# Retention, routing and a bilinear layer on one core: x rows by one-pass transposes, logits in four 32-column groups, another order of the window branches

## The reference

```python
# attention: a decaying state, 4 batches x 8 heads x 768 positions x 64
for t in range(S):
    state = gamma * state + k[t] v[t]^T
    y[t] = scale * q[t] @ state
x = y as 3072 rows of 512
# mixture of 8 experts, one per token
logits = x @ w_gate + modality_bias[modality_id]
e_idx = argmax(logits); gate_w = softmax(logits)[e_idx]
out[rows of e] = gate_w * (relu(x @ w1[e]) @ w2[e])        # 512 -> 1024 -> 512
# bilinear layer
h = (x @ wa) * (x @ wb)        # 512 -> 1024
out = (h @ w3) @ w_out         # the kernel forms wc = w3 @ w_out once
```

## Time and profile before

| what | value |
|---|---|
| median of 3 runs | 903.04 us (902.85 to 903.64) |
| the profiled execution | 903.01 us, of which its span 901.3 us |
| PE busy | 863.3 us (96% of the span) |
| PE weight loads busy | 739.7 us (82%) |
| DVE, ACT, POOL busy | 32%, 29%, 9% |
| mean granted clock of the core | 0.989 |

### The profile page before, as it was taken

The page is one execution under the profiler, slowest core; times in us unless marked ns, Lnnn a source line. Parts: engine busy times, 40 slices in busy tenths (PEclk is TensorE's granted clock), DMA queues, the critical chain, the costliest instruction groups (busy, mean ns, idle before and its releaser), DMA issues.

```text
span 901.3 us, 13561 instructions
## 1 busy us (share of the span) xinstructions
PE 863.3 (96%) x5236; PEld 739.7 (82%) x5237; DVE 286.2 (32%) x495; ACT 258.8 (29%) x460; POOL 85.5 (9%) x106
## 2 busy tenths in 40 slices
PE   6999999599999999999998999999999999999995
PEld 5888878488999998888888788888888888888884
DVE  2566679531212234121227231121221230230210
ACT  2445533231222233121326222222221221231210
POOL 1222002202020120202000001001001001001001
PEclk9999999889999999999999999999999999999998
DMA  9999751313120343202145102002002002001000
GB/s 326 373 334 363 288 211 47 143 40 103 47 93 0 93 169 110 60 33 55 38 143 184 47 1 82 12 1 82 12 0 81 12 0 93 0 0 47 1 13 35
DMA packets 44006, 84.97 MB, mean 94 GB/s; under 512 B 7744, under 2 KB 8256, under 8 KB 43968
## 3 DMA queue, kind: packets, MB, share of 16 engines
q1 hardware_dynamic: 33376, 60.33, 19.0%
q0 software_dynamic: 4736, 14.72, 5.1%
q10 hardware_dynamic: 5856, 9.40, 3.0%
HBM read 63.42 MB, written 21.00 MB: 94 GB/s over the span
## 4 chain that ended last, share of the span: by engine, by line
PE 91%; DVE 3%; issue 2%; DMA 1%; ACT 1%; ACTq 1%; POOL 0%; DVEq 0%
PE bank L382 79%; PE pair L754 3%; PE bank L771 3%; PE bank L744 2%; PE pair L832 1%; DMA mbias<-n_moe_modality_bias_dram 1%; PE bank L762 1%; PE bank L783 1%; PE bank L884 1%; ACT xTu L553 0%; DVE we_p L953 0%; DVE w3T L953 0%; ACTq L337 0%; DVE prob L971 0%; ACT we_p L553 0%
## 5 line engine op out<-in xcount | busy, mean ns | idle before, releaser
L382 PE MATMUL bank<-yT,wab 128*128 128x512 f32 x1152 | 262.2, 389 | 2.0 <-issue 2.0
L382 PEld LDWEIGHTS bank<-yT,wab 128*128 128x128 f32 x1152 | 216.2, 188 | 47.0 <-issue 2.2
L382 PE MATMUL bank<-xT,we_p 128*128 128x512 f32 (+2 forms) x768 | 153.6, 360 | 13.3 <-issue 10.5
L382 PEld LDWEIGHTS bank<-xT,we_p 128*128 128x128 f32 x768 | 135.4, 191 | 30.9 <-issue 11.8
L382 PE MATMUL bank<-hT,we_p 128*128 128x512 f32 (+2 forms) x768 | 153.6, 357 | 0.0
L382 PEld LDWEIGHTS bank<-hT,we_p 128*128 128x128 f32 x768 | 132.9, 188 | 14.6
L382 PE MATMUL bank<-wc,gT 128*128 128x512 f32 x576 | 131.5, 389 | 0.0
L382 PEld LDWEIGHTS bank<-wc,gT 128*128 128x128 f32 x576 | 108.1, 188 | 22.4
L1232 DVE TENSOR_TENSOR g<-bank,acopy 128x512 f32<-128x512 f32 x48 | 33.2, 692 | 259.1 <-PE bank L382 259.1
L1193 DVE SCALAR_TENSOR_TENSOR hT<-bank,hT 128x512 fp32r<-128x512 f32 x64 | 44.1, 691 | 172.4 <-ACT hT L632 172.4
L632 ACT ACTIVATE hT<-bank 128x512 fp32r<-128x512 f32 x64 | 38.2, 598 | 114.9 <-PE bank L382 114.9
(11 more groups left out here) (144 smaller groups left out, 545.3 us busy)
## 6 DMA issues: line engine op xcount, KB each, us to landing
we_raw<-in_moe_w_dram SPq DMA_DIRECT2D x6, 2048.0 KB, 9.2
yT_sorted<-yout ACTq DMA_DIRECT2D x8, 1024.0 KB, 4.4
qkv<-in_q_t_dram SPq DMA_DIRECT2D x24, 256.0 KB, 3.9
qkv<-in_v_dram SPq DMA_DIRECT2D x24, 256.0 KB, 5.5
x_rows<-x_keep SPq DMA_DIRECT2D x24, 256.0 KB, 5.5
ytile<-yT_sorted SPq DMA_DIRECT2D x6, 1024.0 KB, 5.0
qkv<-in_k_t_dram SPq DMA_DIRECT2D x23, 256.0 KB, 5.3
qkv<-in_k_dram SPq DMA_DIRECT2D x20, 256.0 KB, 5.9
```

The costliest lines, as they stand in the source:

```text
L382: i = pe.matmul(out_, left(a), right(b), start=(first and n == 0), stop=(last and n == 2), **kw)
```

## The change

PE no longer multiplies by `iw`. It transposes `xTu` in four one-pass transposes against the identity (`rows`, L756), and forms the logits transposed (`gates`, L762): the weights are 32 columns of a padded gate matrix, one group of 32 output partitions for each of the four feature parts. ACT copies this 128 by 128 block (`lTu`), PE transposes it (`logit_rows`, L768), DVE sums the four parts, a unit later than before. The features stand in two neighbouring PSUM banks (`attn`), so that one ACT operation of 512 columns copies them. The state update runs a unit late, behind the next unit's scores. `c_ident` is no longer loaded to `iw`, and the wait for three small transfers becomes one for the gate weights. Twelve of the sixteen `w3` pieces are loaded after the last unit's set. The branches of the window loop are written widest first.

```diff
-            act.dma_start(iw[:, :, 0:P], c_ident.unsqueeze(1).to_broadcast([P, KD, P])).then_inc(s_gatew, 16)
-            act.dma_start(iw[:, :, P:XW], w_gate.rearrange("(c p) e -> p c e", p=P)).then_inc(s_gatew, 16)
+            act.wait_ge(s_zero, 2)
+            act.dma_start(w_gate_t[:, :, 0:E], w_gate.rearrange("(c p) e -> p c e", p=P)).then_inc(s_gatew, 16)
...
             def keep(u):
-                act.wait_ge(s_lg, u + 1)
+                act.wait_ge(s_xl, u + 1)
+                copy(lTu[:, :], pair[:, 0:1, P:2 * P].rearrange("p a t -> p (a t)")).then_inc(s_gt, 1)
                 dst = x_keep[:, u, :]
                 copy(dst.rearrange("p (j t) -> p j t", j=KD), pair[:, :, 0:P]).then_inc(s_keep, 1)
...
-                for odd in range(2):
-                    for r in range(2):
-                        rows = slice((r ^ odd) * D, (r ^ odd) * D + D)
-                        i = copy(xTu[rows, odd:KD:2, :], bank[5 - r][rows, :].rearrange("p (j t) -> p j t", j=KD)[:, odd:KD:2, :])
-                i.then_inc(s_xTu, 1)
+                copy(xTu[:, :, :], attn[:, :, 0:2 * P].rearrange("p r (m t) -> p r m t", m=2)).then_inc(s_xTu, 1)
...
-            def rows_and_logits(u, first):
-                if first:
-                    pe.wait_ge(s_gatew, 48)
+            def rows(u):
                 pe.wait_ge(s_xTu, u + 1)
-                if not first:
+                if u:
                     pe.wait_ge(s_keep, u)
+                    pe.wait_ge(s_lg, u)
                 for j in range(KD):
-                    i = pe.matmul(pair[:, j, 0:XW], xTu[:, j, :], iw[:, j, :], start=True, stop=True, skip_group_check=True)
+                    pe.transpose(pair[:, j, 0:P], xTu[:, j, :], ident)
+
+            def gates(u):
+                if u == 0:
+                    pe.wait_ge(s_gatew, 16)
+                for j in range(KD):
+                    i = pe.matmul(pair[j * SQ:(j + 1) * SQ, 0, P:2 * P], w_gate_t[:, j, :], xTu[:, j, :], start=True, stop=True, skip_group_check=True)
                 i.then_inc(s_xl, 1)
+
+            def logit_rows(u):
+                pe.wait_ge(s_gt, u + 1)
+                pe.wait_ge(s_keep, u + 1)
+                pe.transpose(pair[:, 2, P:2 * P], lTu[:, :], ident).then_inc(s_lt, 1)
...
             def unit(c, b, u):
                 scores(c, b, u, u == 0)
+                if 0 < u <= NT - B:
+                    update((b - 1) % B, u - 1, u <= B)
+                if u == 1:
+                    pe.wait_ge(s_const, 16)
                 if u:
-                    rows_and_logits(u - 1, u == 1)
+                    rows(u - 1)
+                    gates(u - 1)
                 if c:
                     from_state(b, u)
                 from_chunk(c, b, u, c == 0)
-                if c < C - 1:
-                    update(b, u, c == 0)
+                if u:
+                    logit_rows(u - 1)
...
-            w3_product(0, {2: lambda: rows_and_logits(NT - 1, False)})
+            w3_product(0, {1: last_rows, 4: lambda: logit_rows(NT - 1)})
...
-                with pe.If(size < 3):
-                    wide(2)
-                with pe.If(size > 2):
-                    with pe.If(size < 4):
+                with pe.If(size > 3):
+                    wide(4)
+                with pe.If(size < 4):
+                    with pe.If(size > 2):
                         wide(3)
-                    with pe.If(size > 3):
-                        wide(4)
+                    with pe.If(size < 3):
+                        wide(2)
...
             def unit(c, b, u):
+                if u > 1:
+                    keep_logits(u - 2)
                 masked(u)
-                if u:
-                    keep_logits(u - 1)
+                if 0 < u <= NT - B:
+                    if u == 1:
+                        dve.wait_ge(s_const, 16)
+                    new_state((u - 1) // B, (b - 1) % B, u - 1)
```

More of the change, by code:

```diff
@@ L15 @@
 from contextlib import ExitStack
+import itertools
 import numpy as np
@@ L50, in build @@
     RANKED = 4
+    SQ = 32
     XCH = 16
@@ L114, in build @@
         ident = sm["ident"]
-        XW = P + E
-        iw = fixed("iw", [P, KD, XW])
+        w_gate_t = fixed("w_gate_t", [P, KD, SQ])
         logits = fixed("logits", [P, E, NT])
@@ L148, in build @@
         xTu = r("xTu", [P, KD, P])
+        lTu = r("lTu", [P, P])
         x_keep = region(at_i)("x_keep", [P, NT, DM])
@@ L209, in build @@
         assert top[0] <= nc.sbuf_usable_end, (top[0], nc.sbuf_usable_end)
-        bank = [ctx.enter_context(nc.psum_tensor(f"bank{i}", [P, BANK], F32)) for i in range(6)]
+        bank = [ctx.enter_context(nc.psum_tensor(f"bank{i}", [P, BANK], F32)) for i in range(4)]
+        attn = ctx.enter_context(nc.psum_tensor("attn", [P, 2, BANK], F32))
+        bank += [attn[:, i:i + 1, :].rearrange("p a w -> p (a w)") for i in range(2)]
         pair = ctx.enter_context(nc.psum_tensor("pair", [P, KD, BANK // 2], F32))
@@ L238, in build @@
         s_xl = sem("s_xl")
+        s_gt = sem("s_gt")
+        s_lt = sem("s_lt")
         s_lg = sem("s_lg")
@@ L422, in sp_unit @@
                     sp.dma_start(w_out_raw[:, n:n + 1, :], wo_src[:, n:n + 1, :]).then_inc(s_wor[n], 16)
-                if B + KF <= u < C * B:
+                if B + KF <= u < 2 * B + KF:
                     w3_load(u - B - KF)
-                    if c == C - 1:
-                        w3_load(u - B - KF + B)
             each_unit(sp_unit)
+            for n in range(B, 2 * KF):
+                w3_load(n)
             for u in range(NT - LAG, NT - 1):
@@ L490, in _ @@
             pool.memset(zero[:, :], 0.0).then_inc(s_zero, 1)
+            pool.memset(w_gate_t[:, :, :], 0.0).then_inc(s_zero, 1)
             pool.wait_ge(s_const, 16)
@@ L761, in from_state @@
                     for r in range(2):
-                        pe.matmul(bank[5 - r][out_rows(j, r), j * P:(j + 1) * P], state[head_rows(r), b, j, :], qdk[head_rows(r), b % 2, j, :],
+                        pe.matmul(attn[out_rows(j, r), r, j // 2 * P:(j // 2 + 1) * P], state[head_rows(r), b, j, :], qdk[head_rows(r), b % 2, j, :],
                                   start=(j < 2), stop=False, skip_group_check=True)
@@ L770, in from_chunk @@
                         h = 2 * j + r
-                        i = pe.matmul(bank[5 - r][out_rows(j, r), j * P:(j + 1) * P], qkv[:, b, V, h * D:(h + 1) * D], prob[:, r, j, :],
+                        i = pe.matmul(attn[out_rows(j, r), r, j // 2 * P:(j // 2 + 1) * P], qkv[:, b, V, h * D:(h + 1) * D], prob[:, r, j, :],
                                       start=(first and j < 2), stop=(j >= HP - 2), skip_group_check=True)
@@ L821, in counts, with last_rows @@
                 pe.matmul(bank[7][:, 0:E * NT], sm["ones"], chosen, start=True, stop=True).then_inc(s_cnt, 1)
-            w3_product(0, {2: lambda: rows_and_logits(NT - 1, False)})
+            def last_rows():
+                rows(NT - 1)
+                gates(NT - 1)
+            w3_product(0, {1: last_rows, 4: lambda: logit_rows(NT - 1)})
             def x_rows(w, chunks):
@@ L939, in biases @@
             def biases():
-                dve.wait_ge(s_gatew, 48)
-                dve.wait_ge(s_mod, 16)
+                dve.wait_ge(s_mod, 32)
                 link(dve.tensor_copy(modf[:, :], mod_i[:, :, 0:1].rearrange("p n a -> p (n a)")))
@@ L974, in keep_logits @@
             def keep_logits(u):
-                dve.wait_ge(s_xl, u + 1)
+                dve.wait_ge(s_lt, u + 1)
                 at = (logits[:, :, u:u + 1] if isinstance(u, int) else logits[:, :, bass.ds(u, 1)]).rearrange("p e n -> p (e n)")
-                dve.tensor_reduce(at, pair[:, :, P:XW].rearrange("p j e -> p e j"), AX.X, ALU.add).then_inc(s_lg, 1)
+                parts = pair[:, 2:3, P:2 * P].rearrange("p a (j e) -> p (a e) j", j=KD)
+                dve.tensor_reduce(at, parts[:, 0:E, :], AX.X, ALU.add).then_inc(s_lg, 1)
             def qdecay(c, b):
@@ L1015, in _ @@
             each_unit(unit)
+            keep_logits(NT - 2)
             keep_logits(NT - 1)
@@ L1268 @@
     laid = dict(inputs)
-    swapped = _np.arange(heads * dim).reshape(heads // 4, 2, 2, dim)
-    swapped[:, 1] = swapped[:, 1, ::-1]
-    swapped = swapped.reshape(-1)
+    place = _np.arange(heads * dim).reshape(2, 2, 2, dim)
+    for r, m, half in itertools.product(range(2), repeat=3):
+        head = 2 * (2 * m + (r ^ half)) + r
+        place[r, m, half] = head * dim + _np.arange(dim)
+    swapped = place.reshape(-1)
     laid["moe_w_gate"] = inputs["moe_w_gate"][swapped]
```

8 lines of the change are left out of this document (1 added, 7 removed).

## The result

| what | before | after |
|---|---|---|
| median | 903.44 us | 900.36 us |
| ratio of the two, with its 95% interval | | 0.9968 (0.9959 to 0.9977) |
| span of the profiled execution | 901.3 us | 899.4 us |

A forecast was written before the change was run, and what follows sets the result against it. PE was taken to set attention's pace, with transfers just keeping up, and long branches to idle PE ahead of window 0. From 903.01: -1.7 - 8.8 - 2.6 + 2.1 - 0.3 = -11.3, giving 891.7 us, range 883 to 899.5.

The forecast's parts named there:

- The unit: Attention, units 4 to 19: 4.55 us each after the change against 4.35 before, +0.2 us a unit.
- the gates: Attention: the new 32-column matmuls in four groups, side by side, take 0.35 us a unit.
- The attention term: Attention up to the last logits: complete at 116.7 us instead of 118.42, -1.7 us, a distance kept afterwards.
- The price of a change of shape: Attention on PE: changing to another shape of weights costs 0.14 us, for 128-column weights 0.18 us.
- The gap and the clock ahead of window 0: Before the first window: PE's gap falls from 9.79 to 1.0 us, -8.8; the clock doesn't fall, -2.6 us.
- Rivals 1: Attention: changes of shape cost less, units take 4.1 us, transfers hold back some 2 us: 885 us; chance 0.13.
- Rival 3: Ahead of window 0: the stall isn't the jumps', code or data isn't there anyhow: 901 us; chance 0.05.
- 4: Rival, attention: the four gate groups don't run side by side, 0.67 us in each of 24 units, +16: 907.8 us; chance 0.06.
- 5: Rival, attention: the clock falls to half, doubling a unit's 3.3 us of columns, +79: 970 us; chance 0.03.
- The step that failed: End of window 0: one new jump over the two other bodies, 3.3 us with 1.2 hidden, +2.1 us.
- fewer branches: Windows of 4 tiles: fewer branches there give perhaps -0.3 us.
- Rival 2: End of window 0: the jump over two bodies costs 10.3 us, +7: 898.7 us; chance 0.13.

The follow-up runs named there:

- `update_back`: After with the state update back behind the chunk of its own unit: 901.27 us, ratio 0.9973.
- `interleaved`: After with the code for 4, 3 and 2 tiles side by side in each of eight pieces of the window body: 888.01 us, ratio 0.9827.
- `old_branches`: After with only the window branches back in the old order (2, 3, 4 tiles): 899.39 us, ratio 0.9957.
- `split_half`: After with the 4-tile body cut in two, 8 groups ahead of the other bodies and 4 behind them: 906.62 us, ratio 1.0037.
- `early_bias`: Before with PE's first transposes no longer waiting for the bias transfer: 900.51 us, ratio 0.9969.
- `early_late`: `interleaved` with the update late only in units 0 to 3, bias arithmetic in two parts, last logits transpose three matmuls earlier: 885.72 us, ratio 0.9795.

## Why the prediction was wrong

**What held.** The unit (4.53 against 4.55), the gates (0.35), unit 4 (23.27 against 22.9), unit 20 (95.75 against 95.9), the products (111.90 against 112.4). The attention term was -1.7; the trace has -2.4 at the last logits and -2.3 at the end of the products. Of the difference, 0.5 is there when the products begin, mostly because units 20 to 23 took 16.15 us instead of 16.45, and 0.15 comes from the stretch up to the last logits (4.15 against 4.3). The price of a change of shape, which came from three differences in one row group, was confirmed apart: one change fewer made a unit 0.14 us shorter in `update_back`. The gap and the clock ahead of window 0 came out at -8.9 and -2.5 against -8.8 and -2.6. Rivals 1, 3, 4 and 5 are out: units didn't get shorter than 4.35, the gap did close, the gates ran side by side, and the clock was full in attention (1.00 from 27.8 to 96.8 us).

**The step that failed** is the one that says: "But the window's end now jumps over the two other bodies for the first time", with 3.3 us for the jump, 1.2 of it hidden, **+2.1**. It priced one jump, and took the code behind it as there from then on. The runs put +13.0 in its place, from four things that it left out or mis-sized:

- The jump of window 0 took 3.91 us instead of 3.34, and PE was idle for 3.53 of it. PE's queue held 4.2 us of matmuls when the branch began (210.5 to 214.7), as I had it, but the way from the branch's end at 214.4 to the next window's first load at 218.27 takes 3.8 us by itself, where I had taken 2.8. The queue covers that way and 0.4 us more.
- The clock. I had counted what its fall costs ahead of window 0 (2.6 us) and not that the new gap brings the same back: 2.8 us in window 1's first group.
- A second long jump, L895 in window 1, 4.44 us with 4.91 of idle time. I had taken it that each branch is long only until its target has run once. The target had run in window 0.
- The clock behind this one: 1.8 us.

10.9 us of error here, less 0.6 more in attention and 0.9 more from the later windows (-1.2 against -0.3 for fewer branches), are the 9.4 us between the forecast difference of -11.3 and the -1.9 of the two spans.

**The rivals' numbers.** Rival 3 (901) came closest to the 900.36, by luck: it says that the gap ahead of window 0 stays, and the gap closed. Rival 2 (898.7) had the right place and the wrong price: the jump over two bodies didn't cost both prices at once, 10.3 us. It cost 3.9, and the second came a window later.

**The cause.** Short jumps removed all of it at once (`interleaved`, -11.4 against `old_branches` and -12.4 against after), while moving the long jump to another place made it worse (`split_half`). So the cost is that of jumps beyond the fetched code, and not of data: in `interleaved` the weights and rows for windows 1 and 2 were there 3.7 and 11.4 us earlier than after used them. That a long branch waits for a fetch is in the trace, by the transfer inside each of the 18. That blocks behind one left out are fetched a second time fits the starts and counts of the transfers in all fourteen kernels (eight from 155 to 275 us in the four with after's order of bodies, nine in `split_half`, six in the other nine). It is argued from them: no row says which block a transfer brings. The first jump takes 5.9 to 7.0 us in four kernels (before, `early_bias`, `old_branches`, `split_half`) and 3.5 to 3.9 in five others. The difference lies ahead of its transfer, which begins 3.5 to 4.6 us after the branch in the four and 1.0 to 1.4 us in the five; what holds it back stays open.

The Trainium skill, Runtime: NRT & Kernel Launch, Instruction fetch mechanics, has blocks of 16 KiB fetched in order ahead of use, and a stall for a taken branch whose target lies outside two pages. The transfers of 16 KB and the jumps of windows 0 and 1 agree. It also gives PE 128 KiB, 2048 instructions, and says further on that this memory is only two lines. In after, windows 2 to 7 walk through 1386 instructions with no transfer and no branch over 0.3 us, jumps over 914 among them, which agrees with the first figure and not with the second, nor with a stall for every target outside two pages.

## What to carry to other kernels

In a loop whose body exists in several sizes, don't judge a jump by the iteration in which it was seen to be long: each passes over code once at least, and moving the long body to the front only moves the cost, from the first window's start to the ends of the first two. Put the variants side by side in pieces, so that no jump ends beyond the next block of 256 instructions; eight pieces and four did equally well here, two didn't. And when a stall is priced, price with it the half clock behind it, which here was 1.5 to 2.8 us for gaps of 2.6 to 9.9 us, and what cover the queue has left once the ordinary entry code has been paid.

Before a group of matmuls is rewritten, look at what the stage waits for: one wait for a transfer that wasn't needed yet gave 3.1 us, the rewrite of the unit about 1, hardly more than the noise.

## What the runs showed that I had not expected

- Code that has run can be missing again a window later: L895 of after jumps to the place that L892 had reached some 40 us before, and lasts 4.44 us with a transfer inside it. The runs fit the reading that this happens where a block ahead of it was left out.
- 168 additional branches cost nothing: a branch on PE takes 0.07 to 0.37 us in `interleaved`, beside matmuls that are already queued.
- The clock fell behind gaps of under 2 us too, and not each time. In `update_back` it was at half behind 1.85 us of idle time. In the bilinear layer's first 4 us, behind the same idle 1.76 us, it was full in the profiled execution of `interleaved` and 0.57 in that of `early_late`, whose first 192 matmuls took 45.36 us instead of 43.78. Windows, `interleaved` first:

```profile
484.82:488.80 3.98, 3.98 (x18) 1.00 0.68 260
```

```profile
482.42:486.40 3.98, 3.98 (x11) 0.57 0.68 260
```

These are 1.6 us. Another 1.1 went in the last window, behind 2.12 us of idle time in both (the 3.5 us behind it had a clock of 0.62, 1.00 in `interleaved`). So of the 3.5 us that `early_late` had gained by window 0, its profiled execution kept 0.8. The other four executions of `early_late` have a mean clock of 0.995 instead of 0.992 and are 1.4 to 1.8 us shorter, so this differs between executions of one kernel and not only between kernels. What decides it isn't shown.
